# The output product of the second FFN in two token halves: 1296 matmuls of 256 columns for 648 of 512

## The reference

```python
for t in range(S):                                  # attention, state (B, H, D, D)
    y[:, :, t] = einsum('bhd,bhde->bhe', q[:, :, t], state)
    v_old = einsum('bhde,bhd->bhe', state, k_n[:, :, t])
    state = state + beta_t * einsum('bhd,bhe->bhde', k_n[:, :, t], v_t - v_old)
x = y as (3072 tokens, 384)
h = maximum(x @ w_in, 0);  x2 = (h * h) @ w_out     # first FFN, 384 -> 2048 -> 384
gate = 1 / (1 + exp(-(x2 @ w_gate)))                # second FFN, 384 -> 1536 -> 384
out = (gate * (x2 @ w_val)) @ w_out2
```

## Time and profile before

| | |
|---|---|
| median of 3 runs | 1011.26 us (1009.72 to 1011.65) |
| the profiled execution's own time | 1009.18 us |
| its span, first to last instruction | 1007.4 us |
| PE busy | 959.8 us (95% of the span), 10030 matmuls |
| PEld busy | 490.9 us (49%), 10030 weight loads |
| DVE busy | 543.9 us (54%) |
| ACT busy | 481.2 us (48%) |
| mean granted clock of TensorE | 0.974 of full speed |

### The profile page before, as it was taken

How to read it: one execution, slowest core, us unless ns; L and a number is a source line. 1 busy time by engine, 2 the same in 40 slices (tenths; PEclk the granted TensorE clock), 3 DMA queues, 4 the chain that set the end, 5 groups by cost and what they waited for, 6 DMA issues and landing times.

```text
span 1007.4 us, 23469 instructions
## 1 busy us (share of the span) xinstructions
PE 959.8 (95%) x10030; PEld 490.9 (49%) x10030; DVE 543.9 (54%) x1075; ACT 481.2 (48%) x865; POOL 13.3 (1%) x27
## 2 busy tenths in 40 slices
PE   2876999999999999999999999999999999999997
PEld 1463565565565456546544444444444444444443
DVE  7979957947857885793335532523423423424322
ACT  4875575756576477555669732232222222221321
POOL 0000000000000000000000000000000000000000
PEclk7868999999999999999999999999999999999999
DMA  9516016015005202202033010010100100100000
GB/s 312 120 35 127 2 34 128 33 49 113 33 4 109 50 34 65 64 33 77 21 126 126 1 63 1 0 62 0 62 0 0 62 0 0 62 0 0 31 0 31
DMA packets 20708, 52.16 MB, mean 52 GB/s; under 512 B 2640, under 2 KB 12880, under 8 KB 20240
## 3 DMA queue, kind: packets, MB, share of 16 engines
q1 hardware_dynamic: 20032, 50.60, 17.8%
q10 hardware_dynamic: 592, 0.33, 0.2%
HBM read 41.48 MB, written 9.44 MB: 51 GB/s over the span
## 4 chain that ended last, share of the span: by engine, by line
PE 87%; DVE 6%; ACT 2%; issue 2%; DMA 1%; SPq 0%; POOL 0%; DVEq 0%; POOLq 0%
PE psum L641 75%; PE psum L555 2%; PE psum L499 1%; PE psum L486 1%; DMA raw_a<-in_w_in 1%; PE psum L512 1%; PE psum L524 1%; DVE attn L1086 1%; PE psum L542 1%; ACT w L822 1%; PE psum L570 1%; PE psum L584 1%; DVE work L1127 1%; PE psum L451 1%; DVE attn L1066 1%
## 5 line engine op out<-in xcount | busy, mean ns | idle before, releaser
L641 PE MATMUL psum<-work,attn 128*128 128x512 f16 x1944 | 419.9, 379 | 0.1
L641 PE MATMUL psum<-work,w 128*128 128x512 f16 x1728 | 386.3, 380 | 9.7 <-issue 5.9
L641 PEld LDWEIGHTS psum<-work,attn 128*128 128x128 f16 x1944 | 190.1, 98 | 229.7 <-DVE work L1127 0.6
L641 PEld LDWEIGHTS psum<-work,w 128*128 128x128 f16 x1728 | 164.2, 98 | 204.5 <-issue 9.5
L728 ACT ACTIVATE work<-work 128x512 f16<-128x512 f32 (+1 forms) x264 | 155.7, 624 | 142.9 <-DVE work L1260 139.9
L1260 DVE SCALAR_TENSOR_TENSOR work<-psum,work 128x512 f32<-128x512 f32 x72 | 49.8, 692 | 271.4 <-PE psum L641 261.8
L728 ACT ACTIVATE work<-psum,scal 128x512 f32<-128x512 f32 x90 | 60.5, 686 | 169.9 <-PE psum L641 169.9
L1108 DVE SCALAR_TENSOR_TENSOR work<-work 128x512 f16<-128x512 f16 x96 | 66.1, 690 | 61.5 <-ACT work L728 59.8
L728 ACT ACTIVATE attn<-psum 64x384 f32<-64x384 f32 (+5 forms) x160 | 65.9, 441 | 65.8 <-PE psum L512 34.7
L728 ACT ACTIVATE work<-psum 128x512 f32<-128x512 f32 x96 | 57.2, 595 | 64.3 <-PE psum L641 63.0
L1066 DVE TENSOR_TENSOR attn<-attn 128x31 f32<-128x31 f32 (+15 forms) x186 | 63.8, 343 | 6.4
(11 more groups left out here) (97 smaller groups left out, 558.5 us busy)
## 6 DMA issues: line engine op xcount, KB each, us to landing
attn<-in_kt SPq DMA_DIRECT2D x24, 192.0 KB, 4.2
attn<-in_v SPq DMA_DIRECT2D x24, 192.0 KB, 4.6
attn<-in_kn SPq DMA_DIRECT2D x24, 192.0 KB, 3.8
x_spill<-work SPq DMA_DIRECT2D x6, 768.0 KB, 3.4
xt<-x_spill SPq DMA_DIRECT2D x6, 768.0 KB, 5.0
y_out<-work SPq DMA_DIRECT2D x6, 768.0 KB, 3.6
attn<-in_qt SPq DMA_DIRECT2D x20, 192.0 KB, 4.1
work<-in_w_out SPq DMA_DIRECT2D x1, 3072.0 KB, 23.7
```

The costliest lines, as they stand in the source:

```text
L641: m = mm(dst, x, z, start=first and i == 0, stop=last and i == len(a) - 1)
```

## The change

`project2` no longer issues, for each output bank, three matmuls over the 512 tokens, but three over the first 256 tokens and then three over the last 256. The weights are the same, and are loaded again for the second half. Nothing else of the kernel is altered: waits, slots, banks and the loop stay.

```diff
                 for j in range(KC):
                     hi, lo = (w[:, k, P * j:P * (j + 1)] for w in (wl_hi, wl_lo))
-                    last = product3(o_bank[j], (hi, lo, hi), (h_hi[:, k % SLOTS], h_hi[:, k % SLOTS], h_lo[:, k % SLOTS]),
-                                    k == 0, k == N2 - 1)
+                    for half in range(2):
+                        at = slice(TOK // 2 * half, TOK // 2 * (half + 1))
+                        last = product3(o_bank[j][:, at], (hi, lo, hi),
+                                        (h_hi[:, k % SLOTS, at], h_hi[:, k % SLOTS, at], h_lo[:, k % SLOTS, at]),
+                                        k == 0 and half == 0, k == N2 - 1 and half == 1)
                 last.then_inc(gslot_free, 1)
```

## The result

| | before | after |
|---|---|---|
| median of 13 runs each | 1011.85 us (1009.72 to 1014.03) | 1013.53 us (1011.41 to 1014.77) |
| ratio, 95% interval | | 1.0017 (1.0009 to 1.0025) |
| the profiled execution's own time | 1009.18 us | 1014.77 us |
| its span | 1007.4 us | 1013.0 us |
| matmuls, and as many weight loads | 10030 | 10678 |

The change makes the kernel slower by 1.7 us, 0.17%. The interval leaves zero out, and its middle lies under the 0.2% that the prediction named as what a measurement can tell from no change.

The account below looks back on a forecast made before the run. The second FFN was taken as bound by the PE stream: 139.86 us of matmuls removed, 141.48 us added, all else zero, so +1.62 us on the median of 1011.26 us gave 1012.9 us, range 1010.8 to 1017 us.

Parts of the forecast that it names:

- The bound: Second FFN: a pure PE stream, one piece of 418.47 us with 1938 matmuls; DVE and ACT only wait for it.
- (a): Output product's stream: each matmul costs 2.5 ns besides its columns, 109.17 ns at 256 columns; 648 further matmuls add 1.62 us.
- Its rival: Output product's stream: the 2.5 ns don't come per matmul, so no extra cost, 1011.3 us; chance 0.05.
- The f32 transposes: Four short matmuls with full 128x128 weights from 166.09 us, read as 108 ns each, some 1 to 3 ns above their stream.
- (b): Output product: 648 more weight loads, recorded 98 ns each, hidden by the running matmul of 109 ns; cost nothing.
- The 30 ns of the earlier trace: After an idle stretch, a load at 189.00 us and its matmul some 30 ns later; uncovered, 1296 loads would cost 39 us.
- (c): PE's sequencer: must deliver a load and a matmul per 109 ns; the attention shows 17 ns a pair; nothing added.
- The lead at the jump: PE loop's end: sequencer runs 3 us or 14 matmuls ahead, 1.5 us with narrow ones; still covers the branch's 0.235 us.
- (d): Seam between groups: slack of 1.2 us against DVE grows, as PE moves later by 22.5 ns per block; waits cost zero.
- (e): Output banks: same column rewritten after 109 instead of 216 ns; taken as zero, upper bound 74 us, untested at that distance.
- The Trainium skill's stream of pairs: Load and matmul pairs: about 98 ns at 256 columns, 65 ns more per old matmul, 1053 us; chance 0.01.
- The rival of the instruction store: PE loop grows from 41 to 55 KB; if too large, five jumps back fetch, +5 to +15 us; chance 0.05.

Follow-up runs that it names:

- the two kernels of 1944 further matmuls: Against the kernel before: output product in four parts of 128 tokens, ratio 1.0040; all three products of the second FFN in halves of 256 tokens, ratio 1.0036.
- the run with halves: The changed kernel with two groups written out in the PE loop's body (111 KB): 1017.91 us against 1011.37 us, ratio 1.0069 to the kernel before.
- the two with narrow matmuls: Output product cut finer than in the kernel before: one bank in 16 parts of 32 tokens, 1075.38 us; all banks in parts of 64, 1047.42 us.

## Why the prediction was right

The time of 1012.9 us was forecast, +0.16%; the ratio measured is 1.0017, and the median of 1013.53 us lies in the range. That the medians moved by 1.68 us where 1.62 were forecast is closer than their interval of 0.9 to 2.5 us can show, and so in part luck. What bears the sum out is the stream, and the signs that were named for it: one piece of 2586 matmuls and 420.09 us at clock 1.00, 273 ns for the narrow matmuls, 98 for the loads, 67 blocks. Point by point:

- The bound. The phase was read as a pure PE stream from the one piece of the chain, and so it is: every kernel with a loop of up to 101 KB has one unbroken stream of matmuls, whose length follows from the number and the width of its matmuls.
- (a), the fixed part of 2.5 ns, was the whole sum. Forecast 109.17 ns, measured 109.18; 2.5 ns also with 128 and 64 columns. Its rival (the fixed part belongs to the columns, no cost) falls with the two kernels of 1944 further matmuls, whose intervals leave out zero and hold +4.9 us. That it belongs to the matmul, and not to the load that comes with it, isn't shown. The f32 transposes were a good nearest row: 108 ns read from them.
- (b), loads at no cost, holds down to 64 columns. The margin of 11 ns between 98 and 109 was no margin at all in either direction, since the recorded 98 ns says nothing of what the load holds; at 29 ns spacing it is still recorded as 98. The 30 ns of the earlier trace rows don't hold the array either: pairs came every 29.2 and 25.0 ns.
- (c), the sequencer. Its result holds, its reading doesn't carry far: the attention's 17 ns a pair come from tiles of 64 rows, and full tiles with 32 columns came every 25 ns. The lead at the jump was put at 1.5 us and is 1.7 us.
- (d) and (e), waits and accumulation, cost nothing, (e) down to a distance of 29 ns.
- The Trainium skill's stream of pairs ("TensorE: Matmul & The Clock Gate", "Back-to-back issue gap"), 81 ns at 128 columns and 131 at 512, is contradicted by this kernel's 55.84 and 215.84 ns; the page's other rule, N / 2.4 plus 2.5 ns, is what the runs show.
- The rival of the instruction store had the right mechanism and the wrong place. It was priced at 1 to 3 us for each jump; the holes measured are 1.7 to 3.7 us, and the slow clock after most of them, which the price left out, brings a jump to 2.9 us in the run with halves (5.8 us for two) and, by the medians of the two with narrow matmuls, to about 5. It decides somewhere between 101 and 111 KB, not at 55. The Trainium skill ("Runtime: NRT & Kernel Launch", "Instruction fetch mechanics") has 128 KiB for the PE in one sentence and two lines of 16 KiB, without naming an engine, in another. For the PE the second is ruled out by the kept loops of 41 to 101 KB, and the first is not shown: 111 KB was not kept. Blocks of 16 KB that are only partly used at both ends, and one fetched ahead, could bring the two together, but that is a guess that no run tests.

What failed is the step to the profiled execution. The sum was made against its 1009.18 us and gave 1010.80 for the profile of after, which took 1014.77. 4 us of scatter before the loop were not in the account, and the rows of one execution couldn't show them. Why the first phase scatters so was not tried: by 93 us it had made up 2.1 of the 4.0 us.

## What to carry to other kernels

In an unbroken stream of f16 matmuls count instructions as well as columns: each matmul with its load costs its columns at the granted clock plus 2.5 ns, so halving the width for its own sake costs 2.5 ns for each matmul added, 1.2% of a 512-column matmul, and the weight load beside it is free down to 64 columns. Before a loop body is unrolled or its matmuls are cut finer, count its instructions at 64 bytes each: somewhere between 101 and 111 KB on the PE each jump back begins to stop the engine for microseconds, and in most cases then costs clock. Once the stream has no hole, look at its tail: reading and storing the last banks one by one brought 0.3% here.

## What was not expected of the hardware

- A weight load is recorded with 95 to 98 ns whether matmuls start every 216, 109, 56 or 29 ns. Its length in the profile doesn't say how long it holds the array.
- Pairs of load and full-size matmul with 32 columns came every 25.0 ns, where their columns take 13.3; pairs on tiles of 64 rows side by side came every 17 ns.
- A loop branch whose target is kept takes 0.2 us on the sequencer; one whose target has to be fetched takes 3.4 to 5.1 us. A hole of 3.5 us was followed by a mean granted clock of 0.64 over 4.5 us. The length of the hole alone doesn't decide it: after one of 1.69 us the next 864 matmuls took 140.57 us and after one of 2.06 us 142.27 us, but of two holes of 3.26 and 3.27 us in one kernel the first was followed by a slow stretch and the second wasn't (78.42 and 76.73 us for 864 matmuls).
